# Attention in local tiles of 32 queries by 38 keys, two units a pair, with PV token-major

## What is computed

```python
q_d = q.reshape(B, H, Sd, factor, D).mean(axis=3)      # factor = 4, Sd = 144
out_d = sm_attn(q_d, k_d, v_d)
out_up = np.repeat(out_d, factor, axis=2)
mask = np.abs(pos[:, None] - pos[None, :]) < factor
scores = np.where(mask, scale * np.matmul(q, k.transpose(0, 1, 3, 2)), -1000000000.0)
attn = np.exp(scores - max);  attn = attn / (sum + 1e-09)
out_local = np.matmul(attn, v)
return (out_up + out_local)
```

## Time and profile before

| | us |
|---|---|
| median of 3 runs | 923.59 |
| lowest and highest run | 923.16, 925.59 |
| the profiled execution, its own time | 922.83 |
| its span | 921.1 |
| busy in the span: PE, PEld, DVE, ACT, POOL | 852.1, 727.6, 506.0, 429.7, 210.7 |

### The profile page before, as it was taken

How to read it: one execution, slowest core, us unless ns; L and a number is a source line. 1 busy time by engine, 2 the same in 40 slices (tenths; PEclk the granted TensorE clock), 3 DMA queues, 4 the chain that set the end, 5 groups by cost and what they waited for, 6 DMA issues and landing times.

```text
span 921.1 us, 16050 instructions
## 1 busy us (share of the span) xinstructions
PE 852.1 (93%) x4845; PEld 727.6 (79%) x4846; DVE 506.0 (55%) x1039; ACT 429.7 (47%) x1186; POOL 210.7 (23%) x202
## 2 busy tenths in 40 slices
PE   5787888888999999999999999999699999999994
PEld 3566666667998998998988998998578888888883
DVE  6999999963665565555555555568762111111110
ACT  3777767773555345445445445466053222222221
POOL 2566767643121001001001002000311111111110
PEclk9999999987999999999999999999899999999998
DMA  5555555320100000000000000212060111111110
GB/s 114 145 150 141 146 141 144 95 56 25 47 23 35 1 1 35 0 0 10 24 0 0 34 0 0 90 60 69 35 229 35 46 46 37 42 46 46 38 42 13
DMA packets 88197, 51.57 MB, mean 56 GB/s; under 512 B 64480, under 2 KB 77280, under 8 KB 88160
## 3 DMA queue, kind: packets, MB, share of 16 engines
q1 hardware_dynamic: 85040, 41.16, 16.0%
q0 software_dynamic: 3120, 9.96, 3.2%
HBM read 41.67 MB, written 9.70 MB: 56 GB/s over the span
## 4 chain that ended last, share of the span: by engine, by line
PE 77%; DVE 13%; issue 4%; ACT 2%; SPq 1%; POOL 1%; DVEq 1%; DMA 0%; ACTq 0%; POOLq 0%
PE ps L1443 8%; PE ps L1445 8%; PE ps L1444 8%; PE ps L1333 7%; PE ps L1334 7%; PE ps L1335 7%; PE ps L1309 7%; PE ps L1308 7%; PE ps L1314 7%; DVE ssum L895 3%; DVE smax L885 3%; DVE kdz L870 2%; PE ps L1234 2%; PE ps L1466 2%; PE ps L1350 1%
## 5 line engine op out<-in xcount | busy, mean ns | idle before, releaser
L729 ACT ACTIVATE Eb<-ps 128x384 f32<-128x384 f32 x96 | 47.2, 492 | 145.9 <-PE ps L1314 145.7
L992 DVE TENSOR_SCALAR Tb<-Eb 128x384 f32<-128x384 f32 x96 | 35.4, 369 | 131.1 <-ACT Eb L729 131.1
L659 ACT ACTIVATE prob<-ps,nmax 96x111 f32<-96x111 f32 (+1 forms) x256 | 87.8, 356 | 26.5 <-DVE nmax L889 26.3
L1309 PE MATMUL ps<-xh,WA 128*128 128x384 f32 x288 | 98.5, 342 | 0.0
L1308 PE MATMUL ps<-xh,WA 128*128 128x384 f32 x288 | 97.8, 340 | 0.0
L562 POOL TENSOR_TENSOR xl<-xT,xh 128x384 fp32r<-128x384 f32 x24 | 26.8, 1145 | 280.3 <-ACT xh L701 280.3
L1333 PE MATMUL ps<-WA,gh 128*128 128x512 f32 x216 | 86.8, 402 | 0.2 <-DVE gl L943 0.2
L1335 PE MATMUL ps<-WA,gl 128*128 128x512 f32 x216 | 85.4, 395 | 0.0
L1334 PE MATMUL ps<-WA,gh 128*128 128x512 f32 x216 | 85.2, 394 | 0.0
L738 ACT ACTIVATE Rb<-Tb 128x384 f32<-128x384 f32 x96 | 50.4, 525 | 60.8 <-DVE Tb L994 60.8
L1174 DVE TENSOR_TENSOR hTl<-ps,hTh 128x1024 fp32r<-128x1024 f32 x19 | 23.3, 1224 | 97.6 <-ACT hTh L792 97.6
(11 more groups left out here) (218 smaller groups left out, 2009.1 us busy)
## 6 DMA issues: line engine op xcount, KB each, us to landing
wsraw<-in_moe_w_dram SPq DMA_DIRECT2D x32, 256.0 KB, 3.3
vwin<-in_v_dram SPq DMA_DIRECT2D x32, 166.5 KB
qraw<-in_q_dram SPq DMA_DIRECT2D x32, 144.0 KB, 3.0
kraw<-in_k_dram SPq DMA_DIRECT2D x32, 144.0 KB, 3.1
vdraw<-in_v_dram SPq DMA_DIRECT2D x32, 144.0 KB
y_rows<-yrow SPq DMA_DIRECT2D x6, 768.0 KB, 3.6
wraw<-in_moe_w_in_dram SPq DMA_DIRECT2D x12, 256.0 KB, 5.6
wraw<-in_moe_w_out_dram SPq DMA_DIRECT2D x12, 256.0 KB, 3.4
```

The source lines that it names most:

```text
L659: last = act.activation(prob[0:np_, a.s6, n * w:(n + 1) * w], ps[0:np_, o:o + w], ACT.Exp, scale=sc, bias=nmax[0:np_, a.s6, n:n + 1], accu ...
L1309: pe.matmul(dst, lo, xh[:, kk, :], start=False, stop=False)
```

## The change

A pair has two units in place of three: unit 0 is the pooled attention, unit 1 the whole local attention. NU is 32, and `times_v` comes at lag 3.

- **Local scores.** 18 tiles of 32 queries by 38 keys. Four tiles stand side by side in the 128 partitions of PSUM. One product lays the mask (`band`) under all of them, two small ones (`edge`) correct the first and the last.
- **Softmax.** DVE takes the negated maxima and adds them to the scores in one pass (`shift`); ACT takes one exponential a unit, without a sum; nothing is normalised before PV.
- **PV.** The 18 V tiles stand in `vz`, both heads stacked in 76 partitions, each head's 64 columns in its own block, and two columns of ones that give the sums. The result has tokens in partitions. DVE divides it by the sums (`normalise`), PE turns it back (`turn_back`), and DVE adds it into xT (`add_up`, once a pair). The pooled unit goes the same way, with 65 columns.
- **Loads.** vwin gives way to vz: for each head one DMA of 38 rows of 16 pieces of 256 bytes, and two of 35 rows of one piece for the ends. vdraw has a semaphore of its own (`vd_in`), for which `sum_v` waits.
- **Placement.** All of `copy_turned` and the high part of the slabs go to ACT; q is pooled on POOL, k on DVE. The buffers of probabilities and of pooled q and k are single.
- **Start.** DVE clears vz, pTl, pTd, vd and most of kz before `kz_clear`; POOL waits for that, writes the ones and their masks, and PE waits for all of it (`const_done` 17 in place of 7).

```diff
                 for h in range(2):
                     head = hp * 2 + (n // B * 2 + h)
                     sp.dma_start(vdraw[:, :, h, :, :].rearrange("p c r d -> p c (r d)"),
-                                 vdv[b, head]).then_inc(v_in[par], 16)
-                wait(sp, pv, hp * (B * 3) + (3 * n - 3))
+                                 vdv[b, head]).then_inc(vd_in, 16)
+                wait(sp, pv, hp * (B * 2) + (2 * n - 2))
                 sp.sem_inc(v_due, 1)
+                if static_zero(hp, n):
+                    sp.wait_ge(v_clear, 1)
                 for h in range(2):
                     head = hp * 2 + (n // B * 2 + h)
-                    sp.dma_start(vwin[:, par, :, h, :], v_windows[head + b * H]).then_inc(v_in[par], 16)
+                    own = vz[h * KL:(h + 1) * KL, par, :, h * D:(h + 1) * D]
+                    sp.dma_start(own[:, 1:NL - 1, :], v_inner[head + b * H]).then_inc(v_in[par], 16)
+                    sp.dma_start(own[REACH:KL, 0, :], v[b, head, 0:KL - REACH, :]).then_inc(v_in[par], 16)
+                    sp.dma_start(own[0:KL - REACH, NL - 1, :], v[b, head, S - KL + REACH:S, :]).then_inc(v_in[par], 16)
...
+            pool.wait_ge(kz_clear, 1)
...
+            pool.sem_inc(v_clear, 1)
...
             def sum_v(a):
-                pool.wait_ge(v_in[a.par], a.gen * 64 + 64)
-                wait(pool, pv, 3 * a.p - 5)
+                pool.wait_ge(vd_in, a.p * 32 + 32)
+                wait(pool, pv, 2 * a.p - 1)
...
+            def pool_q(a):
+                pool.wait_ge(turned_out, a.p * ROUNDS + 2)
+                wait(pool, q_pooled, a.p)
+                wait(pool, scored, 2 * a.p - 1)
+                qq = qT[:, a.par, :].rearrange("p (a r) -> p a r", r=FACT)
+                pool.tensor_tensor(qsum[:, :, :], qq[:, :, 0:2], qq[:, :, 2:4], ALU.add).then_inc(q_paired, 1)
+                pool.wait_ge(q_paired, a.p + 1)
+                pool.tensor_tensor(qdT[:, :], qsum[:, :, 0], qsum[:, :, 1], ALU.add).then_inc(q_pooled, 1)
...
             def step(m, dn):
-                a = At(m, dn, NORM)
-                if a.on:
-                    normalise(a)
-                a = At(m, dn, VALUES - 2)
+                a = next_pair(m, dn)
+                if a and dn % 2 == 1:
+                    pool_q(a)
+                a = At(m, dn, 1)
                 if a.on and a.kind == 0:
...
+                act.wait_ge(shifted, a.u + 1)
+                if a.kind == 0:
+                    act.activation(prob_d[:, :, :, :], prob_d[:, :, :, :], ACT.Exp, scale=1.0 / (FACT * FACT)
+                                   ).then_inc(exped, 1)
+                else:
+                    act.activation(prob_l[:, :, :], prob_l[:, :, :], ACT.Exp).then_inc(exped, 1)
...
         def _(dve):
-            dve.memset(kz[:, :, :, :], 0.0)
-            dve.memset(kdz[:, :, :, :], 0.0).then_inc(kz_clear, 1)
+            for h in range(2):
+                for lo in (0, REACH + S):
+                    dve.memset(kz[h * D:(h + 1) * D, :, h, lo:lo + REACH], 0.0)
+                dve.memset(kz[h * D:(h + 1) * D, :, 1 - h, :], 0.0)
+            dve.memset(vd[:, :, :, :], 0.0)
+            dve.memset(pTl[:, :], 1.0)
+            dve.memset(pTd[:, :, :], 1.0)
+            dve.memset(local_parts(NG - 1, 1, slice(0, VC))[D:P], 1.0)
+            dve.memset(vz[:, :, :, :], 0.0).then_inc(kz_clear, 1)
...
+                dve.tensor_reduce(mx, sc, AXX, ALU.max, negate=True).then_inc(maxed, 1)
                 dve.wait_ge(maxed, a.u + 1)
-                wait(dve, exped, a.u - 5)
-                dve.tensor_scalar(nmax[0:np_, a.s6, 0:n], mx, -sc, None, ALU.mult).then_inc(biased, 1)
...
-                dve.tensor_scalar(sm, sm, 1e-9, None, ALU.add).then_inc(summed_eps, 1)
-                dve.wait_ge(summed_eps, a.u + 1)
-                wait(dve, normed, a.u - 5)
-                dve.reciprocal(srec[0:np_, a.s6, 0:n], sm).then_inc(recip, 1)
+                dve.tensor_tensor(pr, sc, wide, ALU.add).then_inc(shifted, 1)
...
+            def normalise(a):
+                dve.wait_ge(pv, a.u + 1)
+                wait(dve, backed, a.u - 1)
+                if a.kind == 0:
+                    out_d = ps[0:QD, DR * BANK:DR * BANK + 4 * (D + 1)].rearrange("p (n c) -> p n c", n=4)
+                    dve.reciprocal(srec_d[:, :], out_d[:, :, D]).then_inc(recip, 1)
+                    dve.wait_ge(recip, 3 * a.p + 1)
+                    dve.tensor_tensor(od_rows[:, :, :].rearrange("p t (h d) -> p (t h) d", h=2), out_d[:, :, 0:D],
+                                      srec_d[:, :].unsqueeze(2).to_broadcast([QD, 4, D]), ALU.mult).then_inc(normed, 1)
+                    return
+                halves = ((0, 3), (3, NG - 3))
+                for first, n in halves:
+                    dve.reciprocal(srec_l[:, first:first + n, :], local_parts(first, n, slice(2 * D, VC))
+                                   ).then_inc(recip, 1)
+                for k, (first, n) in enumerate(halves):
+                    dve.wait_ge(recip, 3 * a.p + 2 + k)
+                    last = dve.tensor_tensor(
+                        ol[:, first:first + n, :].rearrange("p g (h d) -> p g h d", h=2),
+                        local_parts(first, n, slice(0, 2 * D)).rearrange("p g (h d) -> p g h d", h=2),
+                        srec_l[:, first:first + n, :].unsqueeze(3).to_broadcast([P, n, 2, D]), ALU.mult)
+                last.then_inc(normed, 1)
...
-            pe.wait_ge(const_done, 7)
+            pe.wait_ge(const_done, 17)
...
+                            o = (DB + h) * BANK + t * SD
+                            last = pe.matmul(ps[0:QD, o:o + SD], qdT[h * D:(h + 1) * D, t * QD:(t + 1) * QD],
+                                             kdT[h * D:(h + 1) * D, :], start=True, stop=True)
...
-                        dst = ps[0:QT, o + t * TS:o + t * TS + 2 * KW].rearrange("p (h n) -> p h n", h=2)
-                        pe.matmul(dst, identb[0:QT, 0:QT], mask[:, tt, :].unsqueeze(1).to_broadcast([QT, 2, KW]),
-                                  start=True, stop=False)
-                        last = pe.matmul(dst, qT[:, a.par, tt * QT:(tt + 1) * QT],
-                                         kz[:, a.par, :, KSTEP * tt:KSTEP * tt + KW], start=False, stop=True)
+                    pe.matmul(bank(LB, 2 * NG * KL).rearrange("p (n w) -> p n w", n=2 * NG),
+                              sel[:, :, :].rearrange("p a b -> p (a b)"),
+                              band[:, :].unsqueeze(1).to_broadcast([QL, 2 * NG, KL]), start=True, stop=False)
+                    for t in range(NL):
+                        g, c = t // NC, t % NC
+                        o = LB * BANK + g * 2 * KL
+                        dst = ps[c * QL:(c + 1) * QL, o:o + 2 * KL].rearrange("p (h w) -> p h w", h=2)
+                        if t in (0, NL - 1):
+                            pe.matmul(dst, identb[0:QL, 0:QL],
+                                      edge[:, int(t > 0), :].unsqueeze(1).to_broadcast([QL, 2, KL]), start=False, stop=False)
+                        last = pe.matmul(dst, qT[:, a.par, t * QL:(t + 1) * QL],
+                                         kz[:, a.par, :, t * QL:t * QL + KL], start=False, stop=(t >= NL - NC))
                 last.then_inc(scored, 1)
...
+                    pe.wait_ge(v_in[a.par], a.gen * 96 + 96)
+                    for t in range(NL):
+                        g, c = t // NC, t % NC
+                        o = local_out(g)
+                        last = pe.matmul(ps[c * QL:(c + 1) * QL, o:o + VC], pTl[:, t * QL:(t + 1) * QL], vz[:, a.par, t, :],
+                                         start=True, stop=True)
                 last.then_inc(pv, 1)
...
+            def turn_back(a):
+                pe.wait_ge(normed, a.u + 1)
+                if a.kind == 0:
+                    for t in range(2):
+                        o = (DR + 1) * BANK + t * QD
+                        last = pe.transpose(ps[:, o:o + QD], od_rows[:, t, :], ident[0:QD, 0:QD])
+                else:
+                    for g in range(NG):
+                        n, o = rows_of(g), LR * BANK + g * P
+                        last = pe.transpose(ps[:, o:o + n], ol[0:n, g, :], ident[0:n, 0:n])
+                last.then_inc(backed, 1)
...
             def step(m, dn):
-                a = turned_item(m, dn, 0)
-                if a:
-                    turn(a, a.kind)
-                a = At(m, dn, VALUES)
-                if a.on:
-                    times_v(a)
+                done = At(m, dn, VALUES)
+                if done.on:
+                    times_v(done)
+                nxt = next_pair(m, dn)
+                if nxt:
+                    turn(nxt, ROUNDS_AT[dn % 2][0])
                 a = At(m, dn, TURN)
                 if a.on:
                     turn_probs(a)
+                if done.on:
+                    turn_back(done)
                 a = At(m, dn, 0)
                 if a.on:
                     scores(a)
+                if nxt and dn % 2 == 0:
```

(61 more changed lines are left out.)

343 lines of the change are left out of this document (170 added, 173 removed).

## The result

The changed kernel takes **977.5 us** (median of four, 975.9 to 980.3), the kernel before 923.4. The ratio is 1.0589, with a 95% interval of 1.0574 to 1.0604. I had said 947, at most 966. The profiled execution took 977.0 us, with a span of 975.2. The medians and the lowest and highest times given here are of all runs of a kernel, while a ratio leaves out runs that lie more than 1.5% above the fastest of the same kernel.

The account below looks back on a forecast made before the run. V loads on two DMA engines were to bound attention: first vz at 38.4, twelve rounds of 14.0, three of 10.5, then the end, 21.9 us later, plus 1.5 for half clock: 922.83 + 23.4 = 946.2, median 947; range 930 to 966.

Parts of the forecast that it names:

- sum for a round with a slab: Attention, per pair: 8.9 us of vz load plus 5.1 of other traffic make 14.0 us, whatever the compute engines do.
- three rounds behind them: Attention pairs after the last slab: 8.9 us of vz load plus 1.6 for vdraw, 10.5 us each.
- The rest of a round: Attention, a pair's q, k, vdraw and slab traffic: 5.1 us, between 4.2 at 335 GB/s and the old round's 5.5.
- The vz load: Attention, loading V per pair: 8.6 us for the 38-row DMAs at 36 GB/s plus 0.3 for the edges, 8.9 us.
- The reading of two engines: V load: a DMA's rows are dealt equally over at most 16 engines, so 38 rows use two, at 36 GB/s.
- The range: Attention round with a slab 13.1 to 14.5 us; whole kernel 930 to 966 us, meant to leave out 2 in 10.
- The gates at nothing: SP's waits for turned pairs and pv in attention cost nothing; up to 1 us a pair if the cover is gone.
- The compute loop: Attention's program-order chain of turning, scores, PV and normalising: 11.8 us a round (10.3 to 13), hidden under the 14.0 of loads.
- fast rival: Attention: V loads spread well and compute sets the pace at 11.8 us; 914 us (893 to 926), chance 0.12.
- PE too slow: Attention: PE's clock at half in half the stretches makes the loop 15.5 us, total 965 us; chance 0.12.
- The end: After the last vz lands: local PV 1.8, normalise 1.3, turn back 0.5 us, so first_in(1) starts at 241.5.
- The start: Before attention: more clearing makes PE begin at 11.4 us, 6.2 later, and SP's first V load 5.0 later, at 25.3.

Follow-up runs that it names:

- e1: The changed kernel with each head's inner V load of 38 rows issued as two DMAs of 32 and 6 rows: 953.7 us, ratio 1.031.
- e4: The changed kernel with each head's inner V load of 38 rows issued as two DMAs of 37 and 1 rows: 1118.9 us, ratio 1.212.
- e8: The changed kernel with the 32+6 V load split and POOL splitting the slab before summing V: 945.1 us, ratio 1.0235.
- e2: The kernel before with each head's vwin load of 111 rows issued as DMAs of 96 and 15 rows: 896.6 us, ratio 0.971.
- e10: The changed kernel with the 32+6 V load split, POOL's slab split before summing V, and three dense passes before each score stage: 932.8 us.

## Why the prediction was wrong

Direction and mechanism held: the kernel got slower because the load of 38 rows sets the round. What failed is the sum for a round with a slab, 8.9 + 5.1 = 14.0 us, which measured 9.6 + 6.1 = 15.7. Twelve such rounds make 20.5 of the 30.8 us. The other terms were too small as well.

| | forecast | measured | off by |
|---|---|---|---|
| first V load issued | 25.3 | 26.3 | +1.0 |
| twelve rounds with a slab | 14.0 | 15.71 | +20.5 |
| three rounds behind them | 10.5 | 11.33 | +2.5 |
| issue of the last V load to first_in(1) | 16.7 | 20.9 | +4.2 |
| behind first_in(1), against before | +1.5 | +4.1 | +2.6 |
| profiled execution | 946.2 | 977.0 | +30.8 |

**The rest of a round, "I take 5.1".** This is the term that failed most. It measured 6.1 with two engines and 6.0 with one. I had shortened the old round's 5.5 because SP stood in it, and let a rate of 335 GB/s for weights speak for everything; but q, k and vdraw moved at 225 GB/s at full share. 1.0 us a round, 12 us in all.

**The vz load, "8.9".** It measured 9.6. The reading of two engines held (e1 and e4 bear it out), but the 36 GB/s were not steady: 32 from 99 to 102 us. 0.7 a round, 8 us in all.

**The range.** I let the round reach from 13.1 to 14.5 for two terms that were both mere readings across row counts. Their joint error, 1.7, was three times the half microsecond I left for them.

**The gates at nothing.** Right for the changed kernel, where SP waited for no semaphore between 60 and 200 us. The cover was the slow load itself: with it gone (e1), POOL's split behind `sum_v` held the round at some 13.5 us. I had looked only at the turned pairs and pv as SP's gates, and not at w_lo, the semaphore of POOL's slab split.

**The compute loop, 11.8 hidden under 14.0.** Hidden it was. At full clock it is nearer 9.4 (an estimate), at half clock 13.5, so its bounds of 10.3 to 13 missed on both sides. The upper end of my fast rival does not follow from it either: 15 x 1.2 above 914 is 932, and I had written 926. My fast rival would have needed the full clock, which no run kept without added passes, and the gates cut: with the load spread (e1) the kernel still came to 953.7, not 914.

**PE too slow, 0.12.** The clock did fall to half in nearly all of attention, with TensorE busy 24 of 25 us at it. I had argued that the kernel before kept 1.00 at 18% idle; the new passes did not keep it, even where TensorE was never idle (e8). Its price of 15.5 a round was wrong (13.5) and in the rounds it was covered by the loads, but it shows at the end. What keeps the clock down in these narrow passes was not settled.

**The end, "behind the last vz come local PV".** The load was not late: nothing moves from 261 us on, 12.3 us after the issue of the last V load, where I had 13.1. But the last local PV started at 264.67, without waiting for it, for it stands behind first_in(0) in TensorE's list, which ran at half clock from 260.19 on. That is 3.6 us of path that I did not have. PV, normalising and turning back then took 4.9 us (264.67 to 269.62) where I had 3.6. Less the 0.8 of the load, that is the +4.2. Behind first_in(1) the first FFN products cost 1.5, as forecast (the line behind them first runs at 275.70, before at 224.20, so the 50.0 have become 51.5). The other 2.6 arise in the experts, behind 739 us, where nothing was changed; 1.6 of it in the last 16 us, where the granted clock was 0.50 from 959.2 to 962.6 and the kernel before had 1.00 at this place. The rest I did not trace.

**The start.** +1.0 on the first V load. The zeros of vz took 3.96 us; TensorE began at 12.43 where I had 11.4.

**DVE.** In e2's expectation I read 23.8 of 25 us as a bound near 11.3 a round. The round came to 10.2: 27 us lay under a DMA row count in the kernel before.

## What to carry to other kernels

Look at the row count of every DMA in a loop: one that no large number up to 16 divides leaves most engines idle (111 rows, 3 x 37, moved 54 GB/s, 38 rows 32 to 38 and 37 rows 16), and a second DMA for the remainder (96 + 15, 32 + 6) costs an issue and can return 3%. A change that relieves compute is worth nothing while a load sets the round, and when the load is cured, expect the next bounds close behind, here a gate hidden in the order of another engine's list, and the clock. Judge TensorE's clock by the length of a known pass, not by the busy share, and don't take busy time on DVE for work when a tiny instruction is long; look at what POOL does beside it.

## What the runs showed that I had not expected

- TensorE at 40.40 us busy of 40.40 with the granted clock at 0.50 throughout (e8), and at 1.00 for whole stretches when three to six dense 128-row passes of 512 columns were put in front of each score stage, although it then idled more (38.33 of 44.43 us in e10).
- The clock costs these small tiles nearly the full factor: 36 passes of the local PV 2.38 against 1.30 us, 16 of the pooled PV 2.15 against 1.20.
- In pieces of 256 bytes the load of 37 rows moved 16 GB/s and that of 38 rows 32 to 38; at full share q and k (256 bytes too) and vdraw together reached 225 GB/s, the slab with its larger pieces 327.
- A DVE instruction over 72 x 4 elements lasted 1202 ns on average in the kernel before and 166 ns in e2; the long ones end with a POOL pass that runs beside them.
